# Two small VectorE steps of a softmax in a fused attention, mixture-of-experts and rational-MLP kernel: row sums laid out head by head, and the negated bias made by an instruction with two tensor operands

## The chip, the cores and the metric

The kernel runs on one core of one Trainium2 chip. The metric is the device time of one launch in microseconds (us). Three runs of the kernel before took 1002.53, 1002.80 and 1003.68 us; their median is 1002.8 us.

A core has TensorE (PE; matrix products and transposes, results in PSUM), VectorE (DVE), ScalarE (ACT), GpSimd (POOL) and SyncE (SP, which here only issues DMAs). Each engine runs its own instructions in order. Between engines, order is kept by semaphores: `then_inc` on the instruction that produces, `wait_ge` in front of the one that consumes. The kernel also puts such a wait between two VectorE instructions where the second reads what the first wrote.

## The reference

Three layers follow each other. What matters here is the first: attention with a mask by hash buckets.

```python
q_bits = (einsum(q, proj) > 0); k_bits = (einsum(k, proj) > 0)      # 6 bits each
mask   = q_bucket[..., :, None] == k_bucket[..., None, :]
scores = where(mask, q @ k.T / 8, -1e9);  scores -= scores.max(-1)
attn   = exp(scores);  attn /= attn.sum(-1) + 1e-9
out    = attn @ v                     # batch 2, heads 8, seq 768, head_dim 64
```

Its output (1536 tokens of 512) goes into a mixture of 8 experts with the two best chosen for each token, and that into a two-layer network with a rational activation. Neither of the two is touched by the change.

## The kernel before

The 16 heads of the attention are worked as 8 pairs of heads (head A and head B), and each pair in six steps `t` of 128 queries. `pairs` (L350) runs pair 0 on its own, four pairs in a loop of two passes, and the last three unrolled. Each engine's order inside a step is written out by hand in `PE_STEP`, `ACT_STEP` and `DVE_STEP` (L53 to L55):

```python
PE_STEP = ("output", "A scores", 0, "B scores", "A turn", 1, "values", 2, "B turn")
ACT_STEP = (0, 1, "A turned", "A exp", "output", 2, "B exp", "B turned")
DVE_STEP = ("output", 0, "A max", 1, "B max", 2)
```

For one head and one step: TensorE makes the scores into `ps_s[hh]` (L938, L939). VectorE takes the row maximum `mx` (L1216), makes the scale `sc` (L1218), which is zero for a row without a match, and the bias `nb = -mx*sc` (L1221). ScalarE makes `prob = exp(sc*scores + nb)` with the row sum in `rs` (L713; a second small ScalarE instruction reads the sum out). TensorE transposes `prob` into `ps_t` (L947, "turn"), ScalarE copies that to `probT` (L706, "turned"), and TensorE multiplies with `v` (L960, "values"). `ps_t` is shared by the two heads: the turn of head A waits for the copy of head B, and the other way round. The scores of a head wait for the exponential of that head one step before, since `ps_s[hh]` is read by it.

Three steps later VectorE does "output" (`normalise`, L1224): `den = rs + 1e-9` (L1228), `rinv = 1/den` (L1230), and two products of `ps_o` with `rinv` (L1236, L1240).

The numbers 0, 1 and 2 in the orders are points at which the next pair's q and k are prepared. There are eight half-head chunks, each with a "turn" point (TensorE transposes at L913, ScalarE rounds the high part at L739, VectorE subtracts for the low part at L1191 for q or L1194 for k) and a "bits" point (TensorE at L922/L923 or L925/L926 for the hash bits, VectorE at L1205 or L1208 for the comparison). For q the copy `qm` of the high part is made by GpSimd (L569), right after L1191. After the fourth of these copies of a pair GpSimd makes one piece of the first expert's weights (L552, `first_split`: 128 x 1024 from `raw` and `w_r`, all in SBUF). So L552 starts, once per pair, when the last q copy is done; in program order that is beside point 1 of step 3, the row maximum of head B of that step and what follows it.

The tensors `mx`, `sc`, `nb`, `rs`, `den` and `rinv` are small SBUF tiles of 128 partitions.

Of the kernel before, what the change touches and what calls it, by code (L numbers as in the profile page):

```python
# [9 lines left out]
F = mybir.dt.float32  # L10
# [4 lines left out]
ALU = mybir.AluOpType  # L15
# [3 lines left out]
P = 128  # L19
# [3 lines left out]
T = S // P  # L23
# [34 lines left out]
def fused_kernel(nc, q, k, v, proj, w_gate, w_noise, noise, w1, w2, w_in, w_out, a, b, out):  # L58
# [3 lines left out]
    def at(name, off, shape, dt):  # L62
        return nc.alloc_sbuf_tensor_at(name, shape, dt, offset=base + off)
# [28 lines left out]
    def small(name, shape, dt):  # L92
        n = 4 if dt != BF else 2
        for s in shape[1:]:
            n *= s
        t = at(name, c[0], shape, dt)
        c[0] += (n + 31) // 32 * 32
        return t
# [3 lines left out]
    mx = small("mx", [P, 4], F)  # L102
    sc = small("sc", [P, 4], F)
    nb = small("nb", [P, 4], F)
    rs = small("rs", [P, T, 2], F)
    den = small("den", [P, T, 2], F)
    rinv = small("rinv", [P, T, 2], F)

    noise_sb = small("noise_sb", [P, NT, E], F)
# [85 lines left out]
    def sem(name):  # L195
        if name not in sems:
            sems[name] = nc.alloc_semaphore(name)
        return sems[name]
# [18 lines left out]
    soft_ready = [sem("soft_readyA"), sem("soft_readyB")]  # L217
    exp_done = [sem("exp_doneA"), sem("exp_doneB")]
# [5 lines left out]
    den_done = sem("den_done")  # L224
    rinv_done = sem("rinv_done")
# [133 lines left out]
    def o_bank(last, t):  # L359

        return ps_s[0] if last and t == T - 1 else ps_o
# [41 lines left out]
    with nc.Block() as block:  # L403
# [293 lines left out]
        def _(act):  # L697
# [10 lines left out]
            def exp(n, t, hh):  # L708
                act.wait_ge(soft_ready[hh], n * T + t + 1)
                if not (isinstance(n, int) and T * n + t < 2):  # L710
                    act.wait_ge(p_turned[hh], n * T + t - 1)
                i = 2 * (t % 2) + hh
                act.activation(prob[:, hh, t % 2, :], ps_s[hh][:, 0:S], ACT.Exp, bias=nb[:, i:i + 1],  # L713
                               scale=sc[:, i:i + 1], accum_out=rs[:, t, hh:hh + 1]).then_inc(exp_done[hh], 1)

            def o_out(n, t, last):
                act.wait_ge(pv_done, n * T + t + 1)
# [24 lines left out]
            def steps(n, half, par, first, last):  # L742
                for t in range(T):
                    for what in ACT_STEP:
                        if isinstance(what, int):
                            if isinstance(n, int):
                                route_point(n, t, what)
                            if not last:
                                for kind, i in points(t, what):
                                    if kind == "turn":  # L750
                                        round_chunk(n + 1, 1 - par, i)
                        elif what[1:] == " turned" and not (first and t < 1):
                            if not (last and t == T - 1 and what[0] == "B"):
                                turned_out(*back(n, par, t - 1), "AB".index(what[0]))
                        elif what[1:] == " exp":
                            exp(n, t, "AB".index(what[0]))
                        elif what == "output" and not (first and t < 2):
                            m, _, u = back(n, par, t - 2)
                            o_out(m, u, False)
                if last:  # L760
                    turned_out(n, par, T - 1, 1, ps_s[1])
                    o_out(n, T - 2, last)
                    soft(2)
                    o_out(n, T - 1, last)
                    soft(3)
# [401 lines left out]
        def _(dve):  # L1167
# [43 lines left out]
            def softmax(n, t, hh):  # L1211

                i = 2 * (t % 2) + hh
                e = n * T + t + 1
                dve.wait_ge(scored[hh], e)
                dve.tensor_reduce(mx[:, i:i + 1], ps_s[hh][:, 0:S], AX.X, ALU.max).then_inc(row_max_done[hh], 1)  # L1216
                dve.wait_ge(row_max_done[hh], e)
                dve.tensor_scalar(sc[:, i:i + 1], mx[:, i:i + 1], -0.25, SSCALE, ALU.is_gt,  # L1218
                                  ALU.mult).then_inc(scale_done[hh], 1)
                dve.wait_ge(scale_done[hh], e)  # L1220
                dve.tensor_scalar(nb[:, i:i + 1], mx[:, i:i + 1], sc[:, i:i + 1], -1.0, ALU.mult,  # L1221
                                  ALU.mult).then_inc(soft_ready[hh], 1)

            def normalise(n, t, last):  # L1224
                e = n * T + t + 1
                for hh in range(2):
                    dve.wait_ge(exp_done[hh], e)
                dve.tensor_scalar(den[:, t, :], rs[:, t, :], 1e-9, None, ALU.add).then_inc(den_done, 1)  # L1228
                dve.wait_ge(den_done, e)
                dve.reciprocal(rinv[:, t, :], den[:, t, :]).then_inc(rinv_done, 1)  # L1230
                dve.wait_ge(rinv_done, e)
                dve.wait_ge(o_turned, e)
                o = o_bank(last, t)
                share = rinv[:, t, :].rearrange("p (h a) -> p h a", a=1)
                lg_at = lg_head[:, bass.ds(n // (H // 2) * T + t, 1), bass.ds(n % (H // 2) * 2, 2), :]
                dve.tensor_tensor(lg_at.rearrange("p a h e -> p (a h) e"),  # L1236
                                  o[:, 2 * P:2 * P + 4 * E].rearrange("p (h e) -> p h e", h=2),
                                  share.to_broadcast([P, 2, 2 * E]), ALU.mult)
                x_at = x_sb[:, bass.ds(n // (H // 2) * T + t, 1), :, bass.ds(n % (H // 2), 1), :]
                dve.tensor_tensor(x_at.rearrange("p a (h g) b j -> p (a h) g (b j)", h=2),  # L1240
                                  o[:, P:2 * P].rearrange("p (h g j) -> p h g j", h=2, j=P // Q),
                                  rinv[:, t, :].rearrange("p (h a b) -> p h a b", a=1, b=1).to_broadcast([P, 2, Q // 2, P // Q]),
                                  ALU.mult).then_inc(x_done, 1)
# [89 lines left out]
            def steps(n, half, par, first, last):  # L1333
                for t in range(T):
                    for what in DVE_STEP:
                        if what == "A max":
                            softmax(n, t, 0)
                        elif what == "B max":
                            softmax(n, t, 1)
                        elif what == "output" and not (first and t < 3):  # L1340
                            m, _, u = back(n, par, t - 3)
                            normalise(m, u, False)
                        elif isinstance(what, int):
                            point(n, par, t, what, last)
                if last:
                    turned_out(n, T - 2, 1)
                    normalise(n, T - 3, last)
                    turned_out(n, T - 1, 0)
                    logits(*GROUPS[2])
                    add_noise(2)  # L1350
                    best(2)
                    which(2)
                    choose(2)
                    normalise(n, T - 2, last)
                    normalise(n, T - 1, last)
                    logits(*GROUPS[3])
                    place(2)
                    add_noise(3)
                    best(3)
                    which(3)  # L1360
                    choose(3)
                    place(3)
# [7 lines left out]
            def over(z, n, where):  # L1370
# [9 lines left out]
                                          op0=ALU.mult, op1=ALU.add),  # L1380
# [19 lines left out]
                                          op0=ALU.mult, op1=ALU.subtract),  # L1400
                 dve.scalar_tensor_tensor(out=full[:, 2, :], in0=full[:, 0, :], scalar=-float(P), in1=region[:],
                                          op0=ALU.add, op1=ALU.add),
# [166 lines left out]
```

## Time and profile before

| what | value |
|---|---|
| median of three runs | 1002.8 us |
| the profiled execution | 1002.7 us, of which the span of the trace is 1001.1 us |
| attention stage | 0 to about 310 us of the span |
| experts, then rational MLP | about 310 to 722 us, 722 to 1001 us |
| busy over the span: PE, DVE, ACT, POOL | 93%, 59%, 50%, 40% |
| L1221 (`nb`) | 96 instructions, median 214 ns |
| L1228 (`den`) | 48 instructions, median 169 ns, longest 2096 ns |

How to read it: a timeline row gives the start in us from the span's start, the duration in us, the engine, the line of the kernel, the operation, and output <- inputs; in brackets stands the idle time of that engine in front of it and what ended it. A row by source line gives the count and the shortest, median and longest duration in ns. The duration of an instruction includes time in which it has started and cannot go on. Ends of TensorE's products are modelled, so its busy share hides short gaps.

### The profile page before, as it was taken

The page shows a single profiled execution, that of the slowest core. Times are in us where ns is not written, and L with a number is a line of the kernel's source. Part 1 is how long each engine was busy: PE and PEld are TensorE (multiplying, and loading weights), DVE is VectorE, ACT ScalarE, POOL GpSimd, SP SyncE. Part 2 cuts the span into 40 slices and gives each one's busy share as a digit, 9 for nine tenths or more (in the row PEclk, how much of TensorE's full clock was granted, in tenths as well). Part 3 has the DMA queues.
Part 4 walks back from the last instruction along what each step waited for, and adds up shares of the span by engine and source line. Part 5 has one row for each costly group of instructions (what it writes and reads, how often), then busy time and mean ns, then how long its engine had stood idle before and what let it go on. Part 6 is the DMA issues. An engine that isn't in the chain of part 4 may idle for free.

```text
span 1001.1 us, 17998 instructions
## 1 busy us (share of the span) xinstructions
PE 935.4 (93%) x5673; PEld 805.0 (80%) x5674; DVE 592.9 (59%) x1257; ACT 500.7 (50%) x914; POOL 402.9 (40%) x344
## 2 busy tenths in 40 slices
PE   6999999999991899999999999998489999999998
PEld 5788888888871688888888888887379999999997
DVE  6888888888876223222222232221299877878775
ACT  3677777777660222222222222221277777777775
POOL 4401120110243446645563635520577655463222
PEclk9999999999996899999999999999599999999999
DMA  9762423323133867778886768733621110110000
GB/s 203 208 178 55 99 49 81 71 52 87 43 117 128 272 204 246 258 235 246 266 266 207 250 186 275 258 122 105 199 82 50 38 54 22 52 34 9 33 1 31
DMA packets 115476, 134.45 MB, mean 134 GB/s; under 512 B 57186, under 2 KB 75106, under 8 KB 114914
## 3 DMA queue, kind: packets, MB, share of 16 engines
q1 hardware_dynamic: 73778, 63.01, 21.7%
q0 software_dynamic: 19328, 54.53, 17.1%
q10 hardware_dynamic: 22320, 16.26, 5.6%
q8 instruction: 29, 0.48, 0.2%
q14 instruction: 21, 0.17, 0.1%
HBM read 114.12 MB, written 19.66 MB: 134 GB/s over the span
## 4 chain that ended last, share of the span: by engine, by line
PE 81%; DVE 9%; ACT 3%; issue 3%; DMA 1%; POOL 1%; ACTq 0%; another core or an unknown queue 0%; SPq 0%; DVEq 0%; POOLq 0%
PE ps_s L1068 17%; PE ps_o L1093 17%; PE ps_s L1136 13%; PE ps_t L1122 6%; PE ps_t L947 4%; PE ps_o L960 4%; PE ps_s L1122 4%; PE ps_m L1122 3%; PE ps_s L1079 3%; PE ps_s L938 3%; DVE mx L1216 2%; PE ps_s L939 2%; PE ps_m L913 2%; DVE den L1228 1%; PE ps_o L972 1%
## 5 line engine op out<-in xcount | busy, mean ns | idle before, releaser
L534 POOL TENSOR_TENSOR w_r<-raw,w_r 128x1024 f32 (+1 forms) x72 | 171.9, 2403 | 111.9 <-DMA raw<-in_moe_w 48.9
L1068 PE MATMUL ps_s<-w_r,xT 128*128 x744 | 179.6, 398 | 17.0 <-DVE xT L1428 17.0
L1093 PE MATMUL ps_o<-w_r,hT 128*128 x744 | 175.6, 392 | 2.6 <-DVE hT L1432 2.6
L1068 PEld LDWEIGHTS ps_s<-w_r,xT 128*128 128x128 f32 x744 | 139.2, 190 | 45.3 <-issue 17.3
L1093 PEld LDWEIGHTS ps_o<-w_r,hT 128*128 128x128 f32 x744 | 140.8, 189 | 32.1 <-issue 2.8
L1136 PE MATMUL ps_s<-w_r,g_r 128*128 128x512 f32 x576 | 144.0, 395 | 3.8 <-DVE g_r L1514 3.8
L1438 DVE COPY y_sb<-ps_o 128x512 f32<-128x512 f32 x31 | 21.4, 691 | 211.6 <-PE ps_o L1093 211.6
L1136 PEld LDWEIGHTS ps_s<-w_r,g_r 128*128 128x128 f32 x576 | 106.6, 188 | 24.0 <-issue 3.7
L793 ACT ACTIVATE hT<-ps_s 128x1024 fp32r<-128x1024 f32 x31 | 31.8, 1027 | 160.2 <-DVE y_sb L1438 105.8
L654 POOL TENSOR_TENSOR m<-q,g_r 128x384 f32<-128x384 f32 x64 | 65.9, 1030 | 113.2 <-DVE g_r L1502 113.0
L713 ACT ACTIVATE prob<-ps_s,nb,sc 128x768 f32<-128x768 f32 x96 | 95.2, 992 | 23.3 <-DVE nb L1221 22.5
L569 POOL TENSOR_TENSOR qm<-qs,nought 64x384 fp32r<-64x384 f32 x32 | 26.0, 819 | 175.4 <-DVE qs L1191 175.4
L1216 DVE TENSOR_REDUCE mx<-ps_s 128x1 f32<-128x768 f32 x96 | 91.4, 952 | 2.7 <-PE ps_s L939 0.9
L706 ACT ACTIVATE probT<-ps_t 128x768 f32<-128x768 f32 x93 | 74.9, 805 | 29.3 <-PE ps_t L947 29.3
L947 PE MATMUL ps_t<-ident,prob 128*128 128x128 f32 x570 | 79.0, 275 | 0.3 <-DVE probT L1249 0.3
L938 PE MATMUL ps_s<-km,qm 128*128 128x512 f32 x192 | 74.2, 387 | 0.1
L1122 PE MATMUL ps_t<-x2T,w_r 128*128 (+1 forms) x384 | 72.4, 337 | 0.0
L960 PE MATMUL ps_o<-probT,v_in 128*64 128x128 f32 x1128 | 72.0, 277 | 0.0
L1122 PEld LDWEIGHTS ps_t<-x2T,w_r 128*128 128x128 f32 x384 | 68.2, 188 | 2.6
L1480 DVE SCALAR_TENSOR_TENSOR v<-s,ab,t 128x384 f32<-128x384 f32 x64 | 48.7, 761 | 36.2 <-ACT t L848 36.1
L960 PEld LDWEIGHTS ps_o<-probT,v_in 128*64 128x64 f32 x1128 | 60.6, 137 | 9.3 <-issue 8.2
L947 PEld LDWEIGHTS ps_t<-ident,prob 128*128 128x128 f32 x570 | 63.5, 140 | 3.3 <-issue 2.7
(241 smaller groups left out, 1504.7 us busy)
## 6 DMA issues: line engine op xcount, KB each, us to landing
w_r<-in_moe_w POOLq DMA_DIRECT2D x32, 1024.0 KB, 8.5
raw<-in_moe_w SPq DMA_DIRECT2D x56, 512.0 KB, 4.0
xg<-x_slots ACTq DMA_DIRECT2D x124, 64.0 KB, 3.1
y_slots<-y_sb ACTq DMA_DIRECT2D x31, 256.0 KB, 4.5
q_in<-in_q SPq DMA_DIRECT2D x16, 384.0 KB, 4.3
k_in<-in_k SPq DMA_DIRECT2D x16, 384.0 KB, 5.2
raw<-in_moe_w SPq DMA_DIRECT2D x16, 256.0 KB, 4.3
raw<-in_moe_w_in SPq DMA_DIRECT2D x8, 512.0 KB, 5.8
```

The lines of the kernel that those rows point to most:

```text
L534: pool.tensor_tensor(of_chunk(buf, 1, n), raw[:, par, :], of_chunk(buf, 0, n).bitcast(F), ALU.subtract).then_inc(split_done, 1)
L654: pool.tensor_tensor(m2[:], q2[:, f % 2, :], g_r[:, f % 4, 0, :].bitcast(F), ALU.mult).then_inc(m_ready, 1)
L706: act.activation(probT[:, hh, t % 2, :], src[:, 0:S], ACT.Copy).then_inc(pt_ready[hh], 1)
L713: act.activation(prob[:, hh, t % 2, :], ps_s[hh][:, 0:S], ACT.Exp, bias=nb[:, i:i + 1], scale=sc[:, i:i + 1], accum_out=rs[:, t, hh:hh + 1 ...
L938: pe.matmul(o, qm[:, par, hh, rows], km[:, par, hh, c0:c1], start=True, stop=False)
L947: mm = pe.transpose(to[:, u * P:(u + 1) * P], prob[:, hh, t % 2, u * P:(u + 1) * P], ident[:])
L960: mm = pe.matmul(to[64 * hh:64 * hh + 64, 0:P], v_in[:, par, hh, u * D:(u + 1) * D], probT[:, hh, t % 2, u * P:(u + 1) * P], start=(u == 0 ...
L1068: mm = pe.matmul(ps_s[0][:, o * 512:o * 512 + 512], xT[:, par, part, c * P:c * P + P], w_r[:, buf, wpart, col:col + 512], start=(c == 0 an ...
L1093: mm = pe.matmul(ps_o[:, :], hT[:, part, c * P:c * P + P], w_r[:, buf, wpart, col:col + DM], start=(c == 0 and part == 0 and wpart == 0), ...
L1122: mm = pe.matmul(ps_a[f % 4], w_r[:, 0, wpart, c * FF2 + f * P:c * FF2 + f * P + P], x2T[:, par, part, c, :], start=(c == 0 and wpart == 0 ...
L1136: mm = pe.matmul(ps_b[j], g_r[:, f % 4, part, j * P:j * P + P], w_r[:, 1, wpart, f * DM:f * DM + DM], start=(f == 0 and part == 0 and wpar ...
L1216: dve.tensor_reduce(mx[:, i:i + 1], ps_s[hh][:, 0:S], AX.X, ALU.max).then_inc(row_max_done[hh], 1)
```

## The change

Both edits are in the softmax of the attention. `rs` and `den` are laid out as [128, 2, T] in place of [128, T, 2], so the two sums of a step (heads A and B), which lay side by side, lie T = 6 elements apart; `rinv` keeps its layout. And `nb` is made by a `scalar_tensor_tensor` with the number -1.0 as the scalar and both `mx` and `sc` as tensor operands, in place of a `tensor_scalar` with `mx` as the tensor, `sc` as a per-partition scalar and -1.0.

```diff
-    rs = small("rs", [P, T, 2], F)
-    den = small("den", [P, T, 2], F)
+    rs = small("rs", [P, 2, T], F)
+    den = small("den", [P, 2, T], F)
...
-                               scale=sc[:, i:i + 1], accum_out=rs[:, t, hh:hh + 1]).then_inc(exp_done[hh], 1)
+                               scale=sc[:, i:i + 1], accum_out=rs[:, hh, t:t + 1]).then_inc(exp_done[hh], 1)
...
-                dve.tensor_scalar(nb[:, i:i + 1], mx[:, i:i + 1], sc[:, i:i + 1], -1.0, ALU.mult,
-                                  ALU.mult).then_inc(soft_ready[hh], 1)
+                dve.scalar_tensor_tensor(out=nb[:, i:i + 1], in0=mx[:, i:i + 1], scalar=-1.0, in1=sc[:, i:i + 1],
+                                         op0=ALU.mult, op1=ALU.mult).then_inc(soft_ready[hh], 1)
...
-                dve.tensor_scalar(den[:, t, :], rs[:, t, :], 1e-9, None, ALU.add).then_inc(den_done, 1)
+                dve.tensor_scalar(den[:, :, t], rs[:, :, t], 1e-9, None, ALU.add).then_inc(den_done, 1)
                 dve.wait_ge(den_done, e)
-                dve.reciprocal(rinv[:, t, :], den[:, t, :]).then_inc(rinv_done, 1)
+                dve.reciprocal(rinv[:, t, :], den[:, :, t]).then_inc(rinv_done, 1)
```

## Rows read from the trace of the kernel before

**Rows 1.** The stage window view; columns: stretch, length, busy time of each engine (instructions), granted clock.
```profile
120.00:160.00 40.00, 39.45 (x363) 34.06 (x364) 34.24 (x89) 29.82 (x58) 5.62 (x5) 1.00 0.41 95
```

**Rows 2.** The chain of waits from 98 to 192 us, shares of that stretch by line.
```profile
by line: DVE mx L1216 14.1%; PE ps_o L960 10.9%; PE ps_t L947 10.7%; issue 9.4%; PE ps_s L938 7.0%; PE ps_s L939 6.0%; PE ps_m L913 4.7%; DVE den L1228 4.5%; DVE km L1194 3.1%; DVE qs L1191 3.0%; DVE qm L1205 3.0%; PE ps_o L972 2.7%; DVE km
```

**Rows 3.** By source line, the two edited VectorE lines and L1401; ns min/median/max.
```profile
L1228 DVE TENSOR_SCALAR den<-rs x48: 149/169/2096, 36.1 to 306.6; 128x2 f32<-128x2 f32 x48
L1221 DVE TENSOR_SCALAR nb<-mx,sc x96: 212/214/215, 21.1 to 296.8; 128x1 f32<-128x1 f32 x96
L1401 DVE SCALAR_TENSOR_TENSOR full<-full,region x1: 159/159/159, 316.3 to 316.3; 128x8 f32<-128x8 f32 x1
```

**Rows 4.** Timeline of VectorE from 147 us; start us, duration us.
```profile
147.39 0.21 DVE L1221 TENSOR_SCALAR nb<-mx,sc 128x1 f32<-128x1 f32 x1
147.63 0.56 DVE L1205 TENSOR_SCALAR qm<-ps_m 32x384 fp32r<-32x384 f32 x1
148.22 1.22 DVE L1228 TENSOR_SCALAR den<-rs 128x2 f32<-128x2 f32 x1
150.12 0.54 DVE L1194 TENSOR_TENSOR km<-ps_m,kh 64x384 fp32r<-64x384 f32 x1
```

**Rows 5.** Timeline of GpSimd, same stretch.
```profile
146.25 0.82 POOL L569 TENSOR_TENSOR qm<-qs,nought 64x384 fp32r<-64x384 f32 x1 [2.85 <-DVE qs L1191]
147.04 2.38 POOL L552 TENSOR_TENSOR w_r<-raw,w_r 128x1024 f32 x1
```

**Rows 6.** Timeline of ScalarE, same stretch.
```profile
147.64 0.99 ACT L713 ACTIVATE prob<-ps_s,nb,sc 128x768 f32<-128x768 f32 x1 [0.22 <-DVE nb L1221]
149.31 0.49 ACT L739 ACTIVATE kh<-ps_m 128x384 fp32r<-128x384 f32 x1
150.45 0.81 ACT L706 ACTIVATE probT<-ps_t 128x768 f32<-128x768 f32 x1 [0.65 <-PE ps_t L947]
```

**Rows 7.** Timeline of TensorE, same stretch.
```profile
148.79 0.48 PE L938 MATMUL ps_s<-km,qm 128*128 128x512 f32 x1
149.58 0.83 PE L947 MATMUL ps_t<-ident,prob 128*128 128x128 f32 x6
150.71 0.44 PE L925 MATMUL ps_m<-kh,pj 128*128 128x384 f32 x1 [0.30 <-DVE km L1194]
151.26 1.53 PE L960 MATMUL ps_o<-probT,v_in 128*64 128x128 f32 x24
```

**Rows 8.** VectorE L1480 by source line, then timelines of it and GpSimd at 724 us.
```profile
L1480 DVE SCALAR_TENSOR_TENSOR v<-s,ab,t x64: 607/619/2746, 724.3 to 990.1; 128x384 f32<-128x384 f32 x64
724.26 2.75 DVE L1480 SCALAR_TENSOR_TENSOR v<-s,ab,t 128x384 f32<-128x384 f32 x1 [5.19 <-ACT t L848]
724.21 2.38 POOL L534 TENSOR_TENSOR w_r<-raw,w_r 128x1024 fp32r<-128x1024 f32 x1 [5.18 <-DMA raw<-in_moe_w_out]
```

**Rows 9.** Timelines of GpSimd and VectorE, in the first pair.
```profile
46.99 2.38 POOL L552 TENSOR_TENSOR w_r<-raw,w_r 128x1024 f32 x1
48.15 0.21 DVE L1221 TENSOR_SCALAR nb<-mx,sc 128x1 f32<-128x1 f32 x1
```

**Rows 10.** Timelines of GpSimd and TensorE: first and last of the six repeats.
```profile
76.52 2.38 POOL L552 TENSOR_TENSOR w_r<-raw,w_r 128x1024 f32 x1
80.74 1.53 PE L960 MATMUL ps_o<-probT,v_in 128*64 128x128 f32 x24
253.00 2.37 POOL L552 TENSOR_TENSOR w_r<-raw,w_r 128x1024 fp32r<-128x1024 f32 x1
257.62 1.53 PE L960 MATMUL ps_o<-probT,v_in 128*64 128x128 f32 x24
```

**Rows 11.** The view of who waited for whom, 40 to 280 us; us in total, times, longest.
```profile
PE ps_m L925 <- DVE km L1194: 4.1, 8, 1.0
```

**Rows 12.** Timelines of VectorE and GpSimd at 790 us.
```profile
789.93 0.81 DVE L1524 CAST idx_now<-y_pos 128x6 uint32 x1
789.69 1.02 POOL L654 TENSOR_TENSOR m<-q,g_r 128x384 f32<-128x384 f32 x1 [3.22 <-DVE g_r L1502]
```

## The prediction

> **What bounds the kernel now.** I read the windows first. In the attention stage TensorE is busy for 39.45 of 40 us and VectorE for 34.24 of 40 us, with about 30 ns between its 89 instructions [rows 1]: two engines are near their limit, and nothing says yet which ends last. The chain of waits answers that: from 98 to 192 us it runs now along TensorE (L960, L947, L938), now along VectorE (L1216 has 14.1%, L1228 4.5%) [rows 2]. So the two hand the lead to each other, and a delay that stops both moves the end.
>
> By source line the edited instructions look cheap, but L1228 has a median of 169 ns and a longest of 2096 [rows 3]. In the timeline the long one of one pair starts at 148.22, takes 1.22 us and ends at 149.44 [rows 4]; GpSimd's L552 ran from 147.04 to 149.42 [rows 5]. The end of the one is the end of the other: `den`, two elements in and out of SBUF, waits for a running GpSimd instruction. There are eight such waits: this one and five like it (1.22 or 1.23 us), one of 2.10 us and one of 0.65 us in pair 0.
>
> The row to see beside it is `nb` (L1221): it starts at 147.39, inside the same L552, and takes its usual 0.21 us [rows 4, 5]. In its present form it doesn't wait: all 96 take 212 to 215 ns [rows 3]. It has one tensor from SBUF and a per-partition scalar.
>
> **The change part by part.**
>
> *The price of `nb` alone.* The nearest row with two SBUF tensors and a number for the scalar is L1401, 159 ns for 8 elements, against 214 ns now [rows 3]: 55 ns less. This counts only where VectorE leads. L1216 is 14.1% of 94 us of the chain, 13.3 us, so about 14 of its 32 instances there; over 96 that is 42, and 42 x 0.055 = 2.3 us at most, and nothing if TensorE turns out to be right behind. I take the middle, 1.2 us of gain.
>
> *`nb` beside GpSimd.* No row shows a one-element instruction with two SBUF tensors beside GpSimd. The nearest is L1480, same operation, two SBUF tensors of 384 elements: normally 619 ns. At 724.26 it took 2.75 us; GpSimd's L534, as large as L552, ran from 724.21 to 726.59, and L1480 ended at 727.01, 0.42 us after it [rows 8]. So this form waits for the whole GpSimd instruction. `den` shows that an instruction of two elements isn't too small to wait. The bounds are zero (one element never waits) and the rest of L552; I take the rest of L552, as both rows say it. Then `nb` of head B ends at 149.42 + 0.02 = 149.44 and not at 147.60: 1.84 us later. This repeats in every pair, because both are timed by L1191: GpSimd's copy L569 follows it, L552 follows that (146.25, 147.04), and `nb` comes 0.35 us into L552 [rows 4, 5].
>
> The Trainium skill ("SBUF — State Buffer", section "SBUF: two separate sides") says that a VectorE instruction with two SBUF inputs takes a port pair that it shares with GpSimd, exclusively for the whole instruction, against a GpSimd instruction that reads SBUF. Its rule names no smallest size; by it the sum would be the one below, and by an exemption for one element it would be the second rival's. L1480's 2.75 us agree with it; no row here tests one element.
>
> *Who stands behind `nb`.* On ScalarE the exponential of head B starts at 147.64, 0.04 after `nb`, then come the copy of `probT` and the rounding L739 at 149.31 [rows 6]; all move by 1.84. L739 then ends at 149.31 + 1.84 + 0.49 = 151.64, and L1194, which needs it, starts about 151.68 in place of 150.12: VectorE is 1.56 later. On TensorE the scores of head B (148.79) follow that exponential directly and move by 1.84 to 150.63; then the turn of head A (149.58 to 151.42), its copy on ScalarE (150.45 to 152.29), and "values", which started at 151.26 when that copy was ready [rows 6, 7], now at 153.0 to 153.1. L925's own wait of 0.30 us [rows 7] disappears inside this. So all three engines are 1.56 to 1.84 us late at the same place, and none of them has slack left with which to win it back. What VectorE regains is inside these numbers: `den` costs 0.17 in place of 1.22, but qm and `den` now start after 149.44, so it ends near 150.2 and still ahead of L1194.
>
> *`den` itself.* Since `nb` now waits L552 out, `den` meets a free port in all the pairs but the first: its 1.05 us are saved whatever its layout does, and lie under the delay above. In pair 0 L552 at 41.5 us starts after `nb`, and `den` waits 2.10 us. If the new layout saves that, VectorE comes earlier to the `nb` of the next step, and GpSimd, busy without a gap to 49.37, holds that one: `nb` at 48.15 ended at 48.36, and ends at 49.39 either way [rows 9], 1.03 later, and the scores behind it with it. I cost the layout at nothing and pair 0 at +1.05 us.
>
> *The sum.* "Values" comes about 3.6 us after the end of L552 (149.42 to 153.02). For the first of the six repeats that is 78.90 + 3.6 = 82.50 against 80.74, +1.76; for the last 255.37 + 3.6 = 258.97 against 257.62, +1.35 [rows 10]; the six are 1.76, 1.58, 1.76, 1.57, 1.89 and 1.35, together 9.9. By VectorE's L1194 the six give 8.8. With 1.05 for pair 0: 9.8 to 11.0, middle 10.4. Less 1.2 for the shorter `nb`: 9.2 us. The profiled execution took 1002.7 us (span 1001.1), so 1011.9; the median of the runs is 0.1 above it, so **1012.0 us**.
>
> **The rivals.**
>
> *One element doesn't wait, and `den` is freed (faster).* For it: nothing of one element has been seen to wait, `nb` in its old form did not. Against it: two elements do. Then the 1.05 us of `den` go, eight times. But L1194 also waits for ScalarE's L739, ready at 149.80 against L1194's 150.12, so it gains 0.3 here, and "values" waits for the copy that ended at 151.26 [rows 6, 7] and gains 0.1. TensorE's whole wait at L925 is 4.1 us over the eight [rows 11], which is the ceiling; some 2.5 us seem likely, with 1.2 for `nb`: 1002.8 - 3.7 = 999.1 us. It decides from the point at which `nb` stays near 0.16 us beside L552.
>
> *One element doesn't wait, and `den` still does (no change).* That the stride takes `den` off its two-port form isn't shown. L1524 reads a slice of `y_pos` with rows 12 elements apart, and at 789.93 it took 0.81 us and ended at 790.74, when GpSimd's L654 had ended at 790.71 [rows 12]: a strided source waited too. Then only the 1.2 us of `nb` are left: 1001.6 us. The Trainium skill ("Vector Engine (DVE) Microarchitecture Reference", section "Performance modes — why throughput varies by op and dtype") asks for SBUF on both sides and an even count in the outermost dimension, and not for elements side by side; by that rule the new layout changes nothing, and L1524 agrees.
>
> *`nb` waits, but half is regained later.* Between two waits lie steps in which one engine leads and the other might catch up: +4 to +6, 1007 to 1009 us. Against it: all three engines are late together. I count it to the forecast's case.
>
> **How the numbers follow.** `nb` waits: 0.84, of which 0.06 for the case with half regained. `nb` doesn't wait and `den` is freed: 0.09. Neither: 0.07. A measurement of this kernel tells about 0.2%, 2 us, from no change. The forecast's own range: 9.8 - 2.3 = 7.5 at the low end, 11.0 and some 1.5 for short waits elsewhere (beside L569 and L578 in pair 0, and beside GpSimd's scatter issues in the last) at the high end, 1010 to 1015. The range that holds 8 in 10 takes in the lesser case: 1006.5 to 1015. Faster 0.09, the same 0.07, slower 0.84.
>
> **What would show it.** Right: L1221's line with a median near 160 ns and seven instances of about 2 us (one of them 1.2), each ending with an L552; L1228 with no wait of 1.22 us left after pair 0; "values" some 3.6 us after each L552; a period between two L552 of some 36.7 us in place of 35.2. Pair 0 shows the layout: `den` at 41.8 us is 2.1 us long or 0.17. Wrong: L1221 never above 0.25 us. Then the stage doesn't grow, and `den` beside L552 tells which of the first two rivals it is. If L1221 waits as said and the stage grows by less than 7 us, the step that fails is that no engine has slack.

## The result, and the profile after

The changed kernel took 1008.77 us (median of 7 runs, 1008.47 to 1010.96) against 1003.32 us for the kernel before (7 runs beside it, 1001.67 to 1006.82). The ratio is 1.0059, with a 95% interval of 1.0043 to 1.0075: slower by 4.3 to 7.5 us. The forecast was 1012.0 us in a range of 1006.5 to 1015, slower with a chance of 0.84. The profiled execution took 1010.6 us (span 1009.0, against 1001.1).

By source line, after; these answer to [rows 3]:

```profile
L1221 DVE SCALAR_TENSOR_TENSOR nb<-mx,sc x96: 158/159/2090, 20.6 to 304.9; 128x1 f32<-128x1 f32 x96
L1228 DVE TENSOR_SCALAR den<-rs x48: 149/169/2537, 36.2 to 314.7; 128x2 f32<-128x2 f32 x48
```

`nb` is 55 ns shorter at the median, as forecast, and its longest instance is 2090 ns where all 96 were alike. `den` has lost its waits of 1.22 us, and kept one, of 2.54 us. The pair that answers to [rows 4] is here 4 us later. VectorE's timeline (start, duration):

```profile
149.27 0.16 DVE L1221 SCALAR_TENSOR_TENSOR nb<-mx,sc 128x1 f32<-128x1 f32 x1
151.38 2.02 DVE L1221 SCALAR_TENSOR_TENSOR nb<-mx,sc 128x1 f32<-128x1 f32 x1
153.43 0.56 DVE L1205 TENSOR_SCALAR qm<-ps_m 32x384 fp32r<-32x384 f32 x1
154.02 0.17 DVE L1228 TENSOR_SCALAR den<-rs 128x2 f32<-128x2 f32 x1
155.63 0.55 DVE L1194 TENSOR_TENSOR km<-ps_m,kh 64x384 fp32r<-64x384 f32 x1 [0.68 <-ACT kh L739]
```

GpSimd in the same stretch (as [rows 5]):

```profile
150.24 0.82 POOL L569 TENSOR_TENSOR qm<-qs,nought 64x384 fp32r<-64x384 f32 x1 [2.85 <-DVE qs L1191]
151.03 2.36 POOL L552 TENSOR_TENSOR w_r<-raw,w_r 128x1024 f32 x1
```

`nb` starts 0.35 us into L552, as before, and ends at 153.40, where L552 ends at 153.39. `den` then takes 0.17 us. ScalarE (as [rows 6]):

```profile
153.44 0.99 ACT L713 ACTIVATE prob<-ps_s,nb,sc 128x768 f32<-128x768 f32 x1 [2.02 <-DVE nb L1221]
155.11 0.49 ACT L739 ACTIVATE kh<-ps_m 128x384 fp32r<-128x384 f32 x1
156.25 0.81 ACT L706 ACTIVATE probT<-ps_t 128x768 f32<-128x768 f32 x1 [0.65 <-PE ps_t L947]
```

TensorE (as [rows 7]):

```profile
154.13 0.52 PE L913 MATMUL ps_m<-ident,k_in 128*128 128x128 f32 x3 [1.44 <-DVE qm L1205]
154.57 0.50 PE L938 MATMUL ps_s<-km,qm 128*128 128x512 f32 x1
156.24 0.44 PE L925 MATMUL ps_m<-kh,pj 128*128 128x384 f32 x1
156.78 1.53 PE L960 MATMUL ps_o<-probT,v_in 128*64 128x128 f32 x24
```

What is to be seen: the exponential starts when `nb` is free (153.44), L1194 waits for L739 (155.63 is 155.11 + 0.49 and a gap), and "values" (L960) starts at 156.78, 3.39 us after the end of L552; the forecast had 3.6. TensorE stands still in front of L913, a row that the forecast's chain did not have: that transpose at point 0 writes the bank which VectorE's L1205, queued behind `nb`, must first have read. The view of who waited for whom, 40 to 282 us (total us, times, longest), has both waits:

```profile
ACT prob L713 <- DVE nb L1221: 24.8, 35, 2.2
PE ps_m L913 <- DVE qm L1205: 10.5, 7, 1.7
```

All later numbers are for one stretch that every trace has: from the start of the third L552 to the start of the eighth, five pairs with one L552 each inside. It is free of pair 0 and of the stages behind the attention, whose length changes from launch to launch: from the start of the eighth L552 to the end the twelve traces of this document take 740.4 to 750.1 us. Before it is 253.00 - 76.52 = 176.48 us [rows 10]; after it is 260.36 - 78.34 = 182.02, so +5.54 or 1.11 us a pair.

### The profile page after: what moved, and what is told of

The parts are those of the page before. It is cut to its first block, busy times and chain, and to the rows that moved or that the text cites. A ratio compares the mean times of both kernels' runs of the same rounds, so it can differ in the third digit from the quotient of the medians.

```text
span 1009.0 us, 17998 instructions
## 1 busy us (share of the span) xinstructions
PE 934.8 (93%) x5673; PEld 803.3 (80%) x5674; DVE 594.9 (59%) x1257; ACT 500.9 (50%) x914; POOL 403.1 (40%) x344
## 4 chain that ended last, share of the span: by engine, by line
PE 80%; DVE 8%; issue 4%; ACT 4%; POOL 2%; DMA 1%; ACTq 0%; another core or an unknown queue 0%; DVEq 0%; SPq 0%; POOLq 0%
PE ps_s L1068 17%; PE ps_o L1093 17%; PE ps_s L1136 13%; PE ps_t L1122 6%; PE ps_t L947 4%; PE ps_s L1122 4%; PE ps_o L960 3%; PE ps_m L1122 3%; PE ps_s L1079 3%; PE ps_s L938 3%; DVE mx L1216 2%; PE ps_s L939 2%; PE ps_m L913 2%; ACT prob L713 1%; DVE qs L1191 1%
## 5 line engine op out<-in xcount | busy, mean ns | idle before, releaser
L534 POOL TENSOR_TENSOR w_r<-raw,w_r 128x1024 f32 (+1 forms) x72 | 171.9, 2404 | 105.2 <-DMA raw<-in_moe_w 48.2
L569 POOL TENSOR_TENSOR qm<-qs,nought 64x384 fp32r<-64x384 f32 x32 | 26.1, 820 | 183.6 <-DVE qs L1191 183.6
L960 PE MATMUL ps_o<-probT,v_in 128*64 128x128 f32 x1128 | 72.0, 277 | 0.0
L1480 DVE SCALAR_TENSOR_TENSOR v<-s,ab,t 128x384 f32<-128x384 f32 x64 | 48.5, 758 | 36.4 <-ACT t L848 36.2
L960 PEld LDWEIGHTS ps_o<-probT,v_in 128*64 128x64 f32 x1128 | 60.6, 137 | 9.3 <-issue 9.2
```

Source lines behind the costliest of these rows:

```text
L534: pool.tensor_tensor(of_chunk(buf, 1, n), raw[:, par, :], of_chunk(buf, 0, n).bitcast(F), ALU.subtract).then_inc(split_done, 1)
L960: mm = pe.matmul(to[64 * hh:64 * hh + 64, 0:P], v_in[:, par, hh, u * D:(u + 1) * D], probT[:, hh, t % 2, u * P:(u + 1) * P], start=(u == 0 ...
```

## The experiments

The theory: a VectorE instruction with two tensors from SBUF waits for a running GpSimd instruction even when it has one element; two elements with a stride wait as two neighbours do; so `nb` took over the wait from `den`, and holds up three engines where `den` held one. Rivals: the strided layout is slow; or the two-tensor form is slow by itself and the overlap is chance. Each ratio is against the kernel before on the same chip in the same sitting (1003.32 us beside the changed kernel, 999.02 beside the first four experiments, 999.23 beside the next four, 1002.41 beside the last two), so the ratios and differences can be compared, and the times of different sittings cannot.

| run | us | ratio to before, 95% interval | third to eighth L552, us |
|---|---|---|---|
| before | | 1 | 176.48 |
| changed | 1008.77 | 1.0059 [1.0043, 1.0075] | 182.02 |
| layout alone | 998.49 | 1.0000 [0.9987, 1.0014] | 176.54 |
| new `nb` alone | 1006.62 | 1.0083 [1.0060, 1.0107] | 181.87 |
| no `den`, old `nb` | 994.40 | 0.9960 [0.9944, 0.9975] | 173.95 |
| no `den`, new `nb` | 1005.10 | 1.0063 [1.0042, 1.0084] | 181.03 |
| changed, L552 held back | 1000.93 | 1.0019 [1.0004, 1.0033] | 177.90 |
| no `den`, new `nb`, L552 held back | 994.03 | 0.9951 [0.9933, 0.9969] | 171.66 |
| new `nb` for head A alone | 998.44 | 0.9993 [0.9977, 1.0008] | 175.48 |
| bias from the maximum, no `den` | 986.68 | 0.9879 [0.9857, 0.9901] | 168.61 |
| the same with `den` | 995.95 | 0.9932 [0.9910, 0.9953] | 171.48 |
| bias from the maximum, no `den`, again | 988.87 | 0.9859 [0.9836, 0.9883] | 168.66 |

**The layout alone.** The kernel before with the new `rs` and `den` and their four uses; `nb` as it was.

```diff
-    rs = small("rs", [P, T, 2], F)
-    den = small("den", [P, T, 2], F)
+    rs = small("rs", [P, 2, T], F)
+    den = small("den", [P, 2, T], F)
...
```

> The new layout of rs and den alone; nb in its old form. My theory (the slowdown is nb waiting behind GpSimd; two elements six apart still use both ports): no nb above 0.22 us, den still waits about 1.2 us beside L552 once in each pair and longer in pair 0, and the time is that of before within 1.5 us. Rival A (the layout takes den off the two-port form): no den above 0.2 us and 2 to 4 us faster than before. Rival B (the strided layout is what slows the kernel): 5 to 8 us slower than before with nb at 0.21 us.

Measured: no change, 1.0000 [0.9987, 1.0014]. By source line:

```profile
L1221 DVE TENSOR_SCALAR nb<-mx,sc x96: 212/214/217, 20.6 to 294.9; 128x1 f32<-128x1 f32 x96
L1228 DVE TENSOR_SCALAR den<-rs x48: 149/169/1297, 36.5 to 302.7; 128x2 f32<-128x2 f32 x48
```

`den` waits as before, six times 1.21 to 1.23 us after pair 0. So two elements six apart wait for GpSimd just as two neighbours do, and the layout is neither the gain nor the loss. Rivals A and B fall.

**The new `nb` alone.** The kernel before with

```diff
-                dve.tensor_scalar(nb[:, i:i + 1], mx[:, i:i + 1], sc[:, i:i + 1], -1.0, ALU.mult,
-                                  ALU.mult).then_inc(soft_ready[hh], 1)
+                dve.scalar_tensor_tensor(out=nb[:, i:i + 1], in0=mx[:, i:i + 1], scalar=-1.0, in1=sc[:, i:i + 1],
+                                         op0=ALU.mult, op1=ALU.mult).then_inc(soft_ready[hh], 1)
```

> The new form of nb alone; rs and den side by side as before. My theory: seven nb of about 2.0 us, each ending with an L552, no den of 1.2 us after pair 0, and the time of the changed kernel, 5 to 8 us slower than before. Rival B (the layout slows it): the time of before, or 1 to 3 us faster by the shorter nb.

Measured: 7.6 us slower by the medians, 181.87 us over the five pairs.

Its line of `nb`:

```profile
L1221 DVE SCALAR_TENSOR_TENSOR nb<-mx,sc x96: 158/159/2032, 20.6 to 301.6; 128x1 f32<-128x1 f32 x96
```

Six instances of 2.02 or 2.03 us, where seven were expected: in pair 0 the wait fell otherwise, as two of 0.96 and 0.45 us, and `den` waited there for 1.79 us. The whole loss of the change is in this edit: 5.39 us over the five pairs, against 5.54 for both edits.

**Without `den`, with either `nb`.** Two kernels; the addition of 1e-9 is left out and the reciprocal reads `rs`.

```diff
-                dve.tensor_scalar(den[:, t, :], rs[:, t, :], 1e-9, None, ALU.add).then_inc(den_done, 1)
-                dve.wait_ge(den_done, e)
-                dve.reciprocal(rinv[:, t, :], den[:, t, :]).then_inc(rinv_done, 1)
+                dve.reciprocal(rinv[:, t, :], rs[:, t, :]).then_inc(rinv_done, 1)
```

> The kernel before without the instruction den: the reciprocal reads rs, so the addition of 1e-9 is left out. nb in its old form. My theory: no VectorE instruction of the softmax waits behind GpSimd (the reciprocal took 0.17 us beside L569 before); the eight waits on the chain and 48 times about 0.2 us of VectorE go, 3 to 5 us faster than before. If the den waits were wholly hidden by ScalarE's path: under 2 us faster.

> The same without den (the addition of 1e-9 is left out), with nb in its new form. My theory: the nb waits stay as they are, seven of 2.0 us, so it is 2 to 3 us faster than the changed kernel and still 3 to 6 us slower than before; its difference from the run without den and with the old nb is what the new form costs in all, 7 to 10 us. Rival (den and nb share one cost, which one of them pays): about the time of the run with the old nb.

Measured: 4.6 us faster than before with the old `nb`, 6.1 slower with the new, so 10.7 us between them where 7 to 10 were expected. In pair 0 of the second, two `nb` waited, 2.21 and 1.59 us, and not one. The reciprocal, with the same two elements, never waits, not even beside L552; this is its line in the first of the two:

```profile
L1228 DVE RECIPROCAL rinv<-rs x48: 146/165/168, 36.8 to 298.7; 128x2 f32<-128x2 f32 x48
```

Over the five pairs the new form costs 181.03 - 173.95 = 7.08 us when there is no `den` to set off against it. Taking `den` out saves 176.48 - 173.95 = 2.53 us with the old `nb`, where it waits, but 181.87 - 181.03 = 0.84 us with the new, where it doesn't. So the five `den` waits, 5.3 us on VectorE, were worth 1.7 us of time, if the instruction itself is worth the same in both.

**L552 held back.** The changed kernel, and the same without `den`, with GpSimd waiting before L552 until `nb` of head B of step 3 is done:

```diff
+                if not (isinstance(n, int) and n == 0):
+                    pool.wait_ge(soft_ready[1], (n - 1) * T + 4)
                 pool.tensor_tensor(of_first_chunk(1, n), raw[:, par, :].rearrange("p (s n) -> p s n", s=2),
```

> The changed kernel with one wait more: GpSimd starts L552 only when nb of head B of step 3 is done. The forms of nb and den are those of the changed kernel; only what they overlap with is moved. My theory (overlap is what costs, not the form): no nb above 0.25 us after pair 0; L552 then lies over den, which waits about 1.8 us in its place, once in each pair, and ScalarE no longer waits. That gives 176 to 178 us from the third to the eighth L552 (176.5 before, 182.0 in the changed kernel) and a time within 2 us of before. Rival (the two-tensor form of nb, or the strided layout, is slow by itself): the time of the changed kernel.

> The same wait on GpSimd, with nb in its new form and without den (the addition of 1e-9 is left out): nothing of the softmax waits for GpSimd. Its difference from the run without den and with the old nb is the price of the shorter nb alone (55 ns, 96 times). My theory now: the shorter nb is worth more than the 1.2 us of the forecast, since steps without a wait went from 5.87 to 5.80 us in the changed kernel; 2 to 3.5 us less than that run, 171.5 to 172.5 us from the third to the eighth L552 (173.95 there), and 6 to 8 us faster than before. If 1.2 us was right: 173.2 us.

Measured, with `den`: the timeline of VectorE (two lines were added above, so `nb` is L1223, `den` L1230 and L552 is L554).

```profile
149.85 0.16 DVE L1223 SCALAR_TENSOR_TENSOR nb<-mx,sc 128x1 f32<-128x1 f32 x1
150.62 2.01 DVE L1230 TENSOR_SCALAR den<-rs 128x2 f32<-128x2 f32 x1
```

The timeline of GpSimd:

```profile
148.71 0.82 POOL L571 TENSOR_TENSOR qm<-qs,nought 64x384 fp32r<-64x384 f32 x1 [2.85 <-DVE qs L1193]
150.22 2.39 POOL L554 TENSOR_TENSOR w_r<-raw,w_r 128x1024 f32 x1 [0.69 <-DVE nb L1223]
```

The same `nb`, in the same form, takes 0.16 us when L554 starts behind it, and the wait moves to `den`: 2.01 us, to the end of L554 at 152.61. This confirms that the overlap costs the time: the form by itself does not. The five pairs take 177.90 us, so a wait of 2.0 us at `den` costs 4.1 us less over five pairs than one of 2.0 us at `nb`: what counts is who is queued behind. The overall time is 1.7 us above before by the medians, with an interval of 0.4 to 3.3 us, and so below the changed kernel's loss.

Without `den` no instruction of the softmax waits after pair 0: 171.66 us. That gives both prices, if the later start of L552 costs nothing by itself, which no run tests alone. The five `nb` waits cost 181.03 - 171.66 = 9.37 us, 1.87 each, all of what a wait adds to the instruction (2.03 less 0.16). The shorter `nb` alone, against the run with the old `nb` and no `den`, gives 173.95 - 171.66 = 2.29 us for 60 instances: 38 ns of the 55 ns arrive at the end, and over 96 that would be 3.7 us. The whole kernel was 5.2 us faster than before, where 6 to 8 were expected; two `nb` of pair 0, where L552 is not held back, waited 2.37 and 1.59 us.

**Head A alone.** The new form for `hh == 0`, the old form for `hh == 1`, layout as before.

```diff
-                dve.tensor_scalar(nb[:, i:i + 1], mx[:, i:i + 1], sc[:, i:i + 1], -1.0, ALU.mult,
-                                  ALU.mult).then_inc(soft_ready[hh], 1)
+                if hh == 0:
+                    dve.scalar_tensor_tensor(out=nb[:, i:i + 1], in0=mx[:, i:i + 1], scalar=-1.0, in1=sc[:, i:i + 1],
+                                             op0=ALU.mult, op1=ALU.mult).then_inc(soft_ready[hh], 1)
+                else:
+                    dve.tensor_scalar(nb[:, i:i + 1], mx[:, i:i + 1], sc[:, i:i + 1], -1.0, ALU.mult,
+                                      ALU.mult).then_inc(soft_ready[hh], 1)
```

> nb in its new form for head A alone, whose nb comes beside an L552 in no pair but pair 0; head B and the layout as before. My theory: no nb of 2 us after pair 0, den waits 1.2 us as before, half of the shorter nb is won, and the time is 1 to 2 us faster than before. Rival (the form is slow by itself): half of the loss of the changed kernel, 3 us slower.

Measured: 0.8 us faster by the medians, which can't be told from no change; over the five pairs 1.00 us less, 33 ns for each of 30 shorter `nb`, near the 38 ns above, and this without L552 held back. In pair 0 one `nb` of head A met GpSimd all the same and waited, 2.41 us from 44.00. The timeline of VectorE (`nb` of head B is L1225 here, `den` L1232):

```profile
146.77 0.21 DVE L1225 TENSOR_SCALAR nb<-mx,sc 128x1 f32<-128x1 f32 x1
147.60 1.22 DVE L1232 TENSOR_SCALAR den<-rs 128x2 f32<-128x2 f32 x1
```

The timeline of GpSimd:

```profile
146.42 2.37 POOL L552 TENSOR_TENSOR w_r<-raw,w_r 128x1024 f32 x1
```

Head B's `nb` in its old form passes beside L552 in 0.21 us and `den` waits 1.22 us again. What decides is the form of one instruction in six steps, the `nb` that meets L552.

**The bias from the maximum.** Since `sc` is a constant where a row has a match, `nb` needs `mx` alone; a row without a match gets the bias 60 in place of 0, which the division takes out. One tensor from SBUF, two numbers, no wait between `sc` and `nb`; ScalarE waits for both. The 1e-9 is left out in the first of two kernels and kept in the second.

```diff
-                dve.wait_ge(scale_done[hh], e)
-                dve.tensor_scalar(nb[:, i:i + 1], mx[:, i:i + 1], sc[:, i:i + 1], -1.0, ALU.mult,
-                                  ALU.mult).then_inc(soft_ready[hh], 1)
+                dve.tensor_scalar(nb[:, i:i + 1], mx[:, i:i + 1], -SSCALE, 60.0, ALU.mult,
+                                  ALU.min).then_inc(soft_ready[hh], 1)
...
+                act.wait_ge(scale_done[hh], n * T + t + 1)
```

> The version that I expect to be best: nb = min(-mx * scale, 60) by a tensor_scalar with two numbers, one tensor from SBUF, no use of sc, so no wait between sc and nb; no den (the addition of 1e-9 is left out; it is below the rounding of a row sum of at least 1). For a row without a match the bias is 60 in place of 0, which the division takes out again. ScalarE waits for sc as well. My theory: no nb above 0.2 us beside L552, as one SBUF tensor doesn't wait; about 154 ns each; 171 to 172.5 us from the third to the eighth L552, 6 to 9 us faster than before and about equal to the run with the wait on GpSimd and without den. Rival: any shorter nb brings a wait.

> The bias from the maximum alone, as in the run before this one (60 in place of 0 for a row without a match), with den kept as in the kernel before. It parts the two halves of that run's gain. My theory: den waits 1.2 us beside L552 again, or 1.4 us, since nb ends earlier; from the third to the eighth L552 some 2 to 3.5 us more than the 168.6 us without den, so 170.5 to 172, and 6 to 9 us faster than before. If removing den was the whole gain: the time of before.

> The version without den and with the bias from the maximum alone once more (1e-9 left out, 60 in place of 0 for a row without a match), beside the last on the same chip: 168.6 us from the third to the eighth L552 as before, and about 12 us faster than the kernel before.

Measured: 1.2% and 1.4% faster than the kernel before in two sittings, the fastest of all. The timeline of VectorE in the first (`mx` is L1217 here, `sc` L1219, `nb` L1221, the reciprocal L1228):

```profile
140.16 0.96 DVE L1217 TENSOR_REDUCE mx<-ps_s 128x1 f32<-128x768 f32 x1
141.15 0.15 DVE L1219 TENSOR_SCALAR sc<-mx 128x1 f32<-128x1 f32 x1
141.22 0.14 DVE L1221 TENSOR_SCALAR nb<-mx 128x1 f32<-128x1 f32 x1
141.98 0.17 DVE L1228 RECIPROCAL rinv<-rs 128x2 f32<-128x2 f32 x1
```

The timeline of GpSimd:

```profile
140.99 2.38 POOL L552 TENSOR_TENSOR w_r<-raw,w_r 128x1024 f32 x1
```

From the end of `mx` (141.12) to the end of `nb` (141.36) pass 0.24 us where it was 0.43 (147.17 to 147.60), and the reciprocal at 141.98 runs beside L552 in 0.17 us. The gain was larger than I expected (168.61 against 171 to 172.5): I had counted the shorter instruction, 144 ns, and not the wait between `sc` and `nb` that goes. That this is the reason is read from the timeline; no run removes that wait alone. By the whole time, 6 to 9 us were expected, and 12.6 and 13.5 were measured. With `den` kept, the stretch takes 171.48 us, so the bias gives 5.0 us and leaving out `den` 2.9; the whole kernel is 6.5 us faster than before, as expected. There `den` waits longer, 1.41 us, since it comes sooner into the same L552:

```profile
L1228 DVE TENSOR_SCALAR den<-rs x48: 149/169/1411, 34.7 to 298.2; 128x2 f32<-128x2 f32 x48
```

The window view from 80 to 240 us (columns as in [rows 1]), first of the kernel before:

```profile
80.00:240.00 160.00, 157.57 (x1446) 135.77 (x1446) 136.41 (x348) 118.11 (x227) 24.10 (x22) 1.00 0.31 71
```

The same window of this one:

```profile
80.00:240.00 160.00, 159.79 (x1495) 141.90 (x1494) 126.00 (x336) 123.29 (x239) 24.93 (x23) 1.00 0.33 77
```

TensorE's weight loads go from 135.77 to 141.90 us: more of its work is done in the same time, and VectorE is less busy, 126.00 against 136.41.

## Why the prediction was right, point by point

**The price of `nb` alone: 55 ns, right; its share of the chain, too small.** I gave it 1.2 us, with the weights of the chain of waits and half of them taken off in case TensorE was right behind. It is worth 2.29 us over five pairs, which makes some 3.7 over all 96 by an estimate from it. That is the term of the sum that was mis-sized, by 2.5 us, and with it the forecast of +9.2 us comes to +6.7, inside the measured 4.3 to 7.5. Where the reasoning failed: I took only instances on VectorE's stretches of the chain. In TensorE's stretches `nb` also stands in a loop of `nb`, exponential and scores that had hardly more slack: in a step that the chain crossed on TensorE, "values" came 5.91 us after the one before (162.16 to 168.07), and in the same step of the changed kernel 5.80 us (167.59 to 173.39). Not every step gains: the one ahead of it took 5.39 us before and 5.40 after. From the first "values" behind L552 to the last one ahead of the next L552, the five steps together took 28.51 us before (151.26 to 179.77) and 28.15 after (156.78 to 184.93). The windows were also read too tightly, though nothing in the sum rests on it: 34.24 us busy of 40 leave 65 ns to each of VectorE's 89 instructions, and not 30.

**`nb` beside GpSimd: right.** 2.02 us, from 151.38 to the end of L552 plus 0.01, against 2.05 in the forecast; seven instances, as said, though all of 2.0 us where one of 1.2 was expected. That one element waits, which no row had shown, is now shown by `nb` and by its reverse in the run with L552 held back. The Trainium skill ("SBUF — State Buffer", section "SBUF: two separate sides") gives no smallest size, and the runs agree: one element waited 2.02 us.

That it is the two tensors from SBUF, and not the operation `scalar_tensor_tensor`, a trace of the kernel before shows. L1492 is the same operation with 384 elements, but one of its two tensors is in PSUM. It began at 727.51, while the second of two L534 ran (726.55 to 729.27), and took 0.62 us, as always (605 to 621 ns in all 48), where L1480, with both tensors in SBUF, had waited beside the first [rows 8]. Its row on VectorE's timeline, then L534 on GpSimd's:

```profile
727.51 0.62 DVE L1492 SCALAR_TENSOR_TENSOR ps_s<-p,ab,ps_s 128x384 f32<-128x384 f32 x1
726.55 2.72 POOL L534 TENSOR_TENSOR w_r<-raw,w_r 128x1024 fp32r<-128x1024 f32 x1
```

**Who stands behind `nb`: right in size, one link missed.** ScalarE's chain was as forecast (exponential 0.04 us after `nb`, L739 1.67 after it, forecast 1.67). On TensorE the scores of head B were held first by L913, and that by L1205 on VectorE, and not by the exponential alone. It made no difference to the size: L1205 ends at 153.99, the exponential's small second instruction at 154.52. "Values" came 3.39 us after L552 in place of 3.6, which is 0.2 us for each of six. A wait cost 1.87 us by the experiments. The forecast's figure was net of `den`: 8.8 to 9.9 us for six, 1.47 to 1.65 each; measured net it is 1.87 - 0.34 = 1.53. So the three engines had no slack, as the prediction said. With the `nb` term a pair came to 182.02 / 5 = 36.4 us; the forecast said some 36.7.

**`den` itself: right, for the reason given.** Its waits went because `nb` waits in front of it, and the layout does nothing: 1.0000 by itself. The rival "one element doesn't wait, and `den` still does" had the second half right; the Trainium skill ("Vector Engine (DVE) Microarchitecture Reference", section "Performance modes — why throughput varies by op and dtype") asks a one-source instruction that uses both read ports for an outermost count that is even (or odd and the same on both sides), and not for neighbours, and the trace of the layout alone agrees, with 1.22 us of wait for two elements six apart. The other rival's saving of some 2.5 us for a freed `den` looks like what its removal gave over the five pairs, 2.53, but that is a coincidence: 0.84 of it is the instruction, and the waits alone gave 1.7.

**Pair 0: the size near, the place wrong.** I had `den` at 41.8 us wait and `nb` of the next step after it. Instead `nb` at 41.05 met L552, which had started at 40.77 and not at 41.50, and `den` waited again. The timeline of VectorE after, then that of GpSimd:

```profile
41.05 2.09 DVE L1221 SCALAR_TENSOR_TENSOR nb<-mx,sc 128x1 f32<-128x1 f32 x1
43.76 2.54 DVE L1228 TENSOR_SCALAR den<-rs 128x2 f32<-128x2 f32 x1
```

GpSimd (the four L569 are one row):

```profile
40.77 2.36 POOL L552 TENSOR_TENSOR w_r<-raw,w_r 128x1024 fp32r<-128x1024 f32 x1 [12.62 <-DMA w_r<-in_moe_w]
43.10 3.17 POOL L569 TENSOR_TENSOR qm<-qs,nought 64x384 fp32r<-64x384 f32 x4
46.24 2.35 POOL L552 TENSOR_TENSOR w_r<-raw,w_r 128x1024 f32 x1
```

At the third L552 the changed kernel was 78.34 - 76.52 = 1.82 us late, where +1.05 less some `nb` gain was forecast. In this pair L552 starts when a load has landed, so the meeting is not fixed by the order of the instructions: the profile with the new `nb` alone has `den` waiting 1.79 us and `nb` 0.96 and 0.45 us there, reaches its third L552 at 76.39 us, and is one of the shortest runs of its kernel (1003.2 us, others up to 1009.97). That this explains the spread of the runs is a guess; it was not tried, and a rival stands beside it: the two shortest runs of that kernel, 1003.2 us both, have mean granted clocks of 0.978 and 0.980 over their whole length, the four longer ones 0.973 to 0.975.

**The numbers.** By the profiled executions the change cost 7.9 us, by the medians 5.5. The profiled execution of the changed kernel is the second longest of its seven and that of the kernel before lies below its median, so the pair of traces shows more than the typical loss: at the start of the eighth L552 it is already 1.82 + 5.54 = 7.36 us. The forecast's 9.2 us lies above both, by the `nb` term and the 0.2 us at "values"; the range of 1006.5 to 1015 us held the median.

## What to carry to other kernels

A cheaper instruction can cost more than a dear one: count the tensors that it reads from SBUF, look in the trace for a VectorE instruction whose end is the end of a GpSimd instruction, and ask the same of any form that you bring in, even for one element. A wait should be priced by what is queued behind it: 2.0 us on `den` cost 4.1 us less over five pairs than 2.0 us on `nb`, since the exponential, the scores and the next rounding hang on `nb`. And before a small instruction is made faster, ask whether it is needed: deriving the bias from one operand and leaving out `den` gave 12.6 us, over twice the 5.5 us that the change lost.

## What was not expected of the hardware

A waiting VectorE instruction didn't always get in at the next end of a GpSimd instruction. In pair 0 `den` started at 43.76 us during four L569 of 0.8 us each that ran back to back from 43.10 to 46.27, and it ended at 46.30, after the last of them: 2.54 us across three ends. The kernel with L552 held back repeats it (2.53 us), so does the `nb` of head A in pair 0 where only head A has the new form (2.41 us from 44.00), and with the new `nb` alone one `nb` waited 0.96 us from 45.46 across one such end. Yet `nb` at 41.05 got in between an L552 and the first L569, and L1480 at 724.26 between two L534 [rows 8]. In all these cases the ends that were passed over lie between two L569, and the ends that let VectorE in are those of L552, of L534 and of the last L569. Why stays open.

The reciprocal, one source, two elements from SBUF to SBUF, never waited beside GpSimd (longest 168 ns in the run without `den`, where it started inside an L552 once in each of six pairs), where the addition with the same operands did.
